# Attention and gated MLP on one core: more products with v in three passes of halves, and a new order of GpSimd's work

## The reference

```python
q_rot, k_rot = rotate(q), rotate(k)          # x1*cos - x2*sin, x1*sin + x2*cos
scores = scale * q_rot @ k_rot.T
scores = scores - max(scores, axis=-1)
attn = exp(scores); attn = attn / (sum(attn) + 1e-9)
x = attn @ v                                 # heads side by side: 2304 x 512
h = x @ w_in                                 # 2304 x 1024
solu = h * softmax(h)
out = (layernorm(solu) * g_ln) @ w_out       # 2304 x 512
```

## Time and profile before

| | us |
|---|---|
| median of 3 runs | 486.35 (486.30 to 486.53) |
| the profiled execution, its own time | 486.43 |
| its span, first to last instruction | 484.6 |
| TensorE busy in the span | 476.6 (98%) |
| VectorE busy | 365.7 (75%) |
| ScalarE busy | 264.2 (55%) |
| GpSimd busy | 195.1 (40%) |
| granted TensorE clock, mean | 1.000 (2.4 GHz throughout) |

### The profile page before, as it was taken

How to read it: one execution, slowest core, us unless ns; L and a number is a source line. 1 busy time by engine, 2 the same in 40 slices (tenths; PEclk the granted TensorE clock), 3 DMA queues, 4 the chain that set the end, 5 groups by cost and what they waited for, 6 DMA issues and landing times.

```text
span 484.6 us, 7699 instructions
## 1 busy us (share of the span) xinstructions
PE 476.6 (98%) x2527; PEld 403.3 (83%) x2527; DVE 365.7 (75%) x578; ACT 264.2 (55%) x397; POOL 195.1 (40%) x240
## 2 busy tenths in 40 slices
PE   8899999999999999999999999999999999999997
PEld 8677888888888888888888878888888888888885
DVE  6867787777778777877776366999997899888731
ACT  4667887778787878877787353033224222322221
POOL 6877446546453745465461012342343121122110
PEclk9999999999999999999999999999999999999999
DMA  8503544545454545445423203133333223322332
GB/s 283 193 17 76 148 148 112 182 126 169 101 165 143 151 133 149 148 112 170 142 72 100 48 25 56 28 66 87 83 68 86 50 49 70 81 54 60 62 78 85
DMA packets 101007, 50.58 MB, mean 104 GB/s; under 512 B 90280, under 2 KB 90280, under 8 KB 99048
## 3 DMA queue, kind: packets, MB, share of 16 engines
q1 hardware_dynamic: 100152, 50.00, 38.6%
q10 hardware_dynamic: 816, 0.10, 0.1%
HBM read 33.33 MB, written 4.79 MB: 79 GB/s over the span
## 4 chain that ended last, share of the span: by engine, by line
PE 95%; DVE 2%; ACT 1%; DMA 1%; issue 0%; ACTq 0%
PE ps L1098 22%; PE ps L1112 20%; PE ps L1126 20%; PE ps L1050 18%; PE ps L1021 8%; PE ps L1065 4%; PE ps L1078 2%; DMA rope<-rope_in 1%; DVE X L735 1%; DVE nm L794 0%; DVE X L740 0%; ACT QK L553 0%; ACT p_main L605 0%; ACT rope L644 0%; ACT QK L568 0%
## 5 line engine op out<-in xcount | busy, mean ns | idle before, releaser
L794 DVE TENSOR_REDUCE nm<-ps 128x1 fp32r<-128x576 f32 x144 | 108.2, 756 | 51.9 <-PE ps L1021 49.3
L1098 PE MATMUL ps<-p_main,V 128*128 128x288 f32 x456 | 129.5, 406 | 0.0
L605 ACT ACTIVATE p_main<-ps 128x576 f32<-128x576 f32 x114 | 74.1, 650 | 40.1 <-PE ps L1050 37.6
L1050 PE MATMUL ps<-QK 128*128 128x288 f32 x320 | 92.9, 371 | 0.8 <-ACT p_main L605 0.5
L394 POOL TENSOR_TENSOR X<-X,rope 128x1152 f32<-128x1152 f32 x26 | 68.6, 2663 | 60.7 <-DVE KB L779 60.5
L1112 PE MATMUL ps<-w_hi,KB 128*128 128x512 f32 x288 | 91.4, 390 | 0.0
L1126 PE MATMUL ps<-w_hi,QK 128*128 128x512 f32 x288 | 90.9, 389 | 0.0
L1098 PEld LDWEIGHTS ps<-p_main,V 128*128 128x128 f32 x456 | 80.3, 190 | 12.2 <-ACT p_main L605 0.2
L1050 PEld LDWEIGHTS ps<-QK 128*128 128x128 f32 x320 | 56.7, 189 | 19.3 <-issue 5.7
L1050 PE MATMUL ps<-KB 128*128 128x288 f32 x320 | 67.7, 293 | 0.0
L626 ACT ACTIVATE X<-ps,neg_max 128x1024 f32<-128x1024 f32 x18 | 20.1, 1118 | 83.3 <-DVE neg_max L839 83.3
(11 more groups left out here) (102 smaller groups left out, 647.6 us busy)
## 6 DMA issues: line engine op xcount, KB each, us to landing
X<-x_in SPq DMA_DIRECT2D x13, 1152.0 KB, 5.1
V<-oe SPq DMA_DIRECT2D x213, 32.0 KB, 1.9
V<-v_in SPq DMA_DIRECT2D x32, 160.0 KB, 2.7
out<-X SPq DMA_DIRECT2D x18, 256.0 KB, 2.3
w_raw<-w_in SPq DMA_DIRECT2D x16, 256.0 KB, 2.9
xT<-x_in SPq DMA_DIRECT2D x2, 1152.0 KB, 10.4
xT<-oe SPq DMA_DIRECT2D x16, 144.0 KB, 2.4
inv<-inv_rows SPq DMA_DIRECT2D x16, 144.0 KB, 3.0
```

The source lines that it names most:

```text
L605: nc.scalar.activation(dst[:, :].rearrange("p (b c) -> p b c", b=2), score_ps[:, :, 0:HALF], ACT.Exp, scale=SCALE).then_inc(exp_done, 1)
L794: nc.vector.tensor_reduce(nm[g][:, at:at + 1], src[:, :, 0:HALF], AX_XY, ALU.max, negate=True)\
L1050: ins = nc.tensor.matmul(score_ps[:, half, 0:HALF], keys[:, of:of + P], queries[:, to + half * HALF:to + (half + 1) * HALF], start=(g == 0 ...
L1098: ins = nc.tensor.matmul(o_ps[a][:, half, 0:HALF], v, p[:, half * HALF:(half + 1) * HALF], start=(k == 0), stop=(k == 9))
```

## The change

`HALVED` becomes `(1, 3, 8)`: head A's second product (k = 1, in pairs 2 to 14), its fourth (as before) and head B's third (k = 8, in pairs 1 to 14) go in three passes. That is 27 more products. Each has its own `v_hi` and `v_lo`; `p_hi` and `p_lo` are shared. Head B's exponentials go through `o_ps[0]`. What makes room for it, or follows from it:

- `take_o(n-1, 1)` moves ahead of `exp(n, 1)`, which now writes into the banks that it empties.
- `second_queries(n+2, 0)` of step 7 leaves ScalarE and goes to GpSimd, behind `add(n+2)`.
- On VectorE `low_p` comes in steps 1, 3 and 7; `low_queries(n+1, 1)` moves from step 1 to 2, and `low_keys(n+2, 0)` from step 7 to 6.
- GpSimd's rotation waits for `low_p` of step 1 instead of `low_queries(n+1, 1)`. After it come `second_queries`, `set_tails`, two `halve_v`, `divide`, and the third `halve_v`.
- In `weigh_halves` the wait for `p_lo` stands ahead of the third pass alone.

```diff
-HALVED = 3
+HALVED = (1, 3, 8)
...
+            def second_queries(m):
+                pool.wait_ge(score_ready, STEPS * (m - 2) + BOTH + 1)
+                nc.gpsimd.tensor_copy(QK[m % 2][other(0), 0, 0:S], x_of(m)[own(0), 1, :]).then_inc(second_done, 1)
+                pool.wait_ge(second_done, m - 2)
...
             for n in range(1, PAIRS):
                 if n + 2 < PAIRS:
-                    pool.wait_ge(low_q_done[1], n + 2)
+                    if n == 1:
+                        pool.wait_ge(low_q_done[1], n + 2)
+                    else:
+                        pool.wait_ge(p_lo_done, halves(n, HALVED[0]))
...
                     rotate(n + 2)
+                if n + 2 < PAIRS:
+                    pool.wait_ge(rot_done, n + 3)
+                    second_queries(n + 2)
+                    set_tails(n + 2)
+                for k in HALVED[0:2]:
+                    if halved(n + 1, k):
+                        halve_v(n + 1, k)
                 if n >= 2:
-                    if n + 2 < PAIRS:
-                        pool.wait_ge(rot_done, n + 3)
                     divide(n - 2)
...
                 for s in range(STEPS):
+                    if s == 1 and n >= 2:
+                        take_o(n - 1, 1)
                     exp(n, s)
...
-                    if s == 1:
+                    if s == 1 and halved(n, HALVED[0]):
+                        low_p(n, HALVED[0])
+                    if s == (2 if halved(n, HALVED[0]) else 1):
                         low_queries(n + 1, 1)
...
-                    if s == 7 and n + 2 < PAIRS:
+                    if s == 6 and n + 2 < PAIRS:
                         low_keys(n + 2, 0)
...
-                for v, p in ((v_hi, p_hi), (v_lo, p_hi), (v_hi, p_lo)):
+                for part, (v, p) in enumerate(((v_hi[i], p_hi), (v_lo[i], p_hi), (v_hi[i], p_lo))):
+                    if part == 2:
+                        pe.wait_ge(p_lo_done, halves(n, k))
```

More of the change, by code:

```diff
@@ L89, in attention_then_mlp @@
         p_lo = sb("p_lo", [P, S], F32R)
-        v_hi = sb("v_hi", [P, P], F32R)
-        v_lo = sb("v_lo", [P, P], F32R)
+        v_hi = [sb(f"v_hi{i}", [P, P], F32R) for i in range(len(HALVED))]
+        v_lo = [sb(f"v_lo{i}", [P, P], F32R) for i in range(len(HALVED))]
         oe = [sb(f"oe{c}", [P, 2, S]) for c in range(2)]
@@ L104, in attention_then_mlp @@
         p_lo_done = sem("p_lo_done")
-        v_hi_done = sem("v_hi_done")
-        v_lo_done = sem("v_lo_done")
+        v_hi_done = [sem(f"v_hi{i}_done") for i in range(len(HALVED))]
+        v_lo_done = [sem(f"v_lo{i}_done") for i in range(len(HALVED))]
+        second_done = sem("second_done")
         x_loaded = [sem(f"x_loaded{c}") for c in range(2)]
@@ L216, in halved, with halves, head, high @@
         def halved(n, k):
-            return k == HALVED and 1 <= n < PAIRS - 1
+            return k in HALVED and (2 if k == HALVED[0] else 1) <= n < PAIRS - 1
+        def halves(n, k):
+            i = HALVED.index(k)
+            return i if n == 1 else 3 * (n - 2) + i + 3
+        def head(k):
+            return k // 5
+        def high(m, a):
+            return m + 4 if a == 0 and m >= 3 else 2 * m + 1
+        def copied(m, a):
+            return m + 4 if a == 0 and m >= 3 else 2 * m + 2
         def last_pair(t):
@@ L472, in _ @@
                 nc.gpsimd.memset(V[c][:, 1, :, 0:D], 1.0).then_inc(v_const, 1)
-            nc.gpsimd.memset(v_hi[:, D:P].bitcast(F32), 1.0).then_inc(v_const, 1)
-            nc.gpsimd.memset(v_lo[:, D:P].bitcast(F32), 0.0).then_inc(v_const, 1)
-            pool.wait_ge(v_const, 6)
+            for i, k in enumerate(HALVED):
+                nc.gpsimd.memset(v_hi[i][:, other(head(k))].bitcast(F32), 1.0).then_inc(v_const, 1)
+                nc.gpsimd.memset(v_lo[i][:, other(head(k))].bitcast(F32), 0.0).then_inc(v_const, 1)
+            pool.wait_ge(v_const, 10)
             nc.gpsimd.memset(expo[:, :], -0.5).then_inc(const_done, 1)
@@ L683, in _ @@
                             second_queries(n + 1, 1)
-                        if s == 1:
-                            take_o(n - 1, 1)
+                        if s == 1 and n == 1:
+                            take_o(0, 1)
                         if s == 2 and n + 1 < PAIRS:
@@ L700, in _ @@
                     if s == (7 if n == 0 else 6) and n + 2 < PAIRS:
-                        high(n + 2, 0)
-                    if s == (8 if n == 0 else 7) and n + 2 < PAIRS:
-                        second_queries(n + 2, 0)
+                        set_high(n + 2, 0)
+                    if n == 0 and s == 8:
+                        second_queries(2, 0)
             take_o(PAIRS - 1, 1)
@@ L802, in row_max, with low_p @@
                     nc.vector.transpose(nm_row[g][:, :], nm[g][:, :].bitcast(F32)).then_inc(turned[g], 1)
[L804 to L807 removed]
+            def low_p(n, k):
+                a = head(k)
+                dve.wait_ge(p_hi_done, halves(n, k))
+                nc.vector.tensor_tensor(p_lo[:, :].rearrange("p (b c) -> p b c", b=2), o_ps[1 - a][:, :, 0:HALF],
                                         p_hi[:, :].bitcast(F32).rearrange("p (b c) -> p b c", b=2), ALU.subtract)\
```

94 lines of the change are left out of this document (51 added, 43 removed).

## The result

The changed kernel takes 500.34 us (median of 5 runs, 500.02 to 501.12) against 486.3 before: 1.0288 times as long, 95% interval 1.0277 to 1.0299. It is 14.0 us slower; 16.8 slower was forecast (503.2, range 484 to 508). The span grew by 14.2, from 484.6 to 498.8.

A forecast was written before the change was run, and what follows sets the result against it. TensorE, busy 98% of the span, was taken to bound the kernel. Products -4.6, rotation +12.0, pair's start +0.3 and +7.0, low_keys +2.1 gave +16.8 on 486.43: 503.2 us, range 484 to 508.

The forecast's parts named there:

- Products: TensorE's 27 products in three passes: each saves 0.17 us, 0.34 a pair, -4.6 in all.
- Rotation: Head B's low_queries wait for GpSimd's rotation half; TensorE waits 1.00 us before step 4 in 12 pairs, +12.0.
- `divide`, with the pair's start: GpSimd's later divide holds head A's low_queries: 0.58 us in each of 12 pairs, +7.0; pair 2 without it, +0.3.
- ScalarE's burst: Queued ScalarE operations at the pair's start delay exp: TensorE loses 0.27, plus 0.03 for low_p; replaced where divide meets low_queries.
- `low_keys`: Moved to step 6, ahead of the row maximum, which comes 0.16 us late with the copy: 13 pairs, +2.1.
- Rival one: VectorE and GpSimd subtractions don't lock each other out: 486.7, or 481.8 to 483 if ScalarE's burst fits; 18%.
- rival two: GpSimd comes first again between the rotation's halves, low_queries wait for both: +31.7, 535 us; 8%.
- rival three: Products in three passes wait for v_hi or p_hi, so steps aren't shorter: 508 us; 2%.
- The signs: Profile after: head B's low_queries about 2.6 us, TensorE waiting about 1 us before step 4, rotation 2.65, steps 2 and 8 1.60.

The follow-up runs named there:

- f3_burst_spread: Changed kernel with head B's low queries on GpSimd, divide behind the add, copy held for low_keys; ScalarE's second_queries moved to step 2, copy_keys to 4: 487.5 us.
- e2_before_early_rot: Kernel before, with only the rotation started earlier in pairs 2 to 13, once step 1's row scores are done: 500.88 us, 1.0296 of before.
- e5_rot_quarters: Changed kernel with the rotation in four multiplications of 128x576 instead of two of 128x1152, starting at the same time: 497.71 us, 1.0235 of before.

## Why the prediction was right

The sign, the mechanism and the place were right, the time within 2.9 us. That it is so near is in part luck, since the two terms that were mis-sized are off in opposite directions.

- **Products, -4.6.** Measured by the marks, -0.37 a pair against -0.34, some -5.
- **Rotation, +12.0.** Too small: +1.29 in step 3 and -0.05 in step 4, 12 x 1.24 = +14.9. The working held to a few hundredths up to the last link: the subtraction ends 3.39 after `low_p` (3.38 forecast), the row maximum 4.19 after it (4.14), step 4's mark would have been due 3.12 after it (3.16). TensorE came 0.22 after the row maximum and not 0.05; that handoff was read from another step, where no second wait lies behind.
- **`divide`, with the pair's start, +7.3.** Steps 0 and 1 give +0.15 a pair, not 0.58. This is the term that was mis-sized most. `divide` was forecast from 1.2 to 2.65 after step 8's mark and runs from 0.74 to 2.17:

```profile
159.52 1.43 POOL L470 TENSOR_TENSOR xT<-xT,inv 128x576 f32<-128x576 f32 x1
...
160.28 1.29 DVE L822 TENSOR_TENSOR KB<-X,QK 64x576 fp32r<-64x576 f32 x1
...
161.49 0.74 DVE L837 TENSOR_REDUCE nm<-ps 128x1 fp32r<-128x576 f32 x1
```

 The failing link is above all the add, which I had ending 0.8 after step 6's mark, held up by VectorE; it starts at 154.24 in this round and ends 0.46 after the mark at 155.13, since VectorE had caught up in step 5. That is 0.34 of the 0.46; the rest is in the round behind it and in the steps. The meeting itself is there, 1.29 for a 0.75 subtraction.
- **ScalarE's burst, 0.27 and 0.03.** In steps 0 to 2 0.17 is lost with or without `divide`, where 0.30 was counted. The cause was half seen: the sum counted ScalarE's operations back to back and left out that `take_o` must wait for TensorE's product. f3_burst_spread shows that this wait sets the `exp` almost as late when the queue has room.
- **`low_keys`, +2.1.** +0.13 a pair in step 7 against 0.16: 1.7.
- **Rival one** (no lock) fell with e2_before_early_rot; **rival two** (GpSimd comes first between its two halves) with the 5.78 us of the rotation and the subtraction's 2.70; **rival three** with the 1.56 and 1.61 of steps 8 and 2.
- The Trainium skill's page SBUF — State Buffer, section "SBUF: two separate sides", was borne out in kind: the loser waits to the end of the instruction it met. Beside the half rotation the subtraction ends 0.6 us after the end of that, and in e5_rot_quarters 0.6 us after the end of a piece half as long. `low_p`, with one input in PSUM, stayed at 745 to 759 ns in all 41 cases, of which 13 lie beside the rotation and 13 beside other work of GpSimd. (Before, too, it was 13: the prediction's "all 14 times" counts the last pair, which has no rotation.)
- **The signs.** `low_queries` of head B at 2.7 us, TensorE's wait for the row maximum, steps 2 and 8 at 1.6 and the second group of long `low_queries` all came. One did not: the rotation was to stay at 2.65 us an operation. The second one's row is 3.17 long, its own wait for VectorE included.

The sum was too high by 5.4 for the pair's start (7.3 against 1.9) and by 0.4 for `low_keys`, and too low by 2.9 for the rotation; it came out 2.8 too high.

## What to carry to other kernels

A wait that no data asks for may keep two engines out of each other's way: before such a wait is dropped or moved, list every VectorE instruction with two SBUF inputs that the GpSimd instruction could then meet, not only the one in view. Where TensorE waits for what comes next on VectorE, the order of two unrelated instructions 0.05 us apart decides half a microsecond; a wait can fix that order, but here it didn't pay, since a late `divide` still got in the way. And a cheaper product is worth its saving only where the chain that feeds it (here `take_o`, `exp`, `p_hi`, `low_p`) has room for a shorter step.

## What the runs showed of the hardware that was not expected

- `w_low`, a VectorE instruction with two SBUF tiles and a scalar per partition, waits for GpSimd as the plain subtraction does: 2.58 us in the place of 0.75.
- Between two GpSimd instructions that need no semaphore, a waiting VectorE instruction comes first: it ends 0.6 us after the first, and the two take 5.78 in the place of 5.28.
- A GpSimd copy of 64x576 (0.66 us) begun 0.04 us ahead is enough to hold VectorE's subtraction for 0.5 us (1.23 in the place of 0.75).
- A second, long given wait behind the one that comes last costs TensorE about 0.1 us (0.22 against 0.12).
